# One change to a sparse-attention and feed-forward kernel: order of the block moves, early weight pieces, and who splits x

## The reference

```
scores = q @ k.T / 8 ; thresh = max(scores, row) - tau
scores = where(scores >= thresh, scores, -1e9)
attn = exp(scores - max) / (sum + 1e-9) ; x = attn @ v        # tokens x 512
h = x @ w_in ; g = max(h, 0) + alpha * min(h, 0) ; x = g @ w_out   # 512 -> 2048 -> 512
out = (((x @ w1) * (x @ w2)) @ w3) @ w_out2                    # 512 -> 1024 -> 1024 -> 512
```

## Time and profile before

| what | value |
|---|---|
| three runs, median (lowest to highest) | 1059.97 us (1058.85 to 1061.64) |
| the profiled execution, own time | 1060.03 us |
| its span in the profile | 1058.1 us |
| busy share PE / DVE / ACT / POOL | 94% / 49% / 40% / 45% |
| attention stage | to about 480 us |
| DMA engines, mean busy share of 150 to 200 us | 0.85 |

### The profile page before, as it was taken

One profiled execution on the slowest core, in us unless ns is written; L12 is line 12 of the kernel. 1 busy time (PEld: TensorE's weight loads), 2 busy tenths in 40 slices (PEclk: granted clock), 3 DMA queues, 4 the chain that ended last, 5 costly groups with the idle time before them and its releaser, 6 DMA issues.

```text
span 1058.1 us, 18205 instructions
## 1 busy us (share of the span) xinstructions
PE 990.3 (94%) x6848; PEld 899.6 (85%) x6848; DVE 519.6 (49%) x1374; ACT 420.0 (40%) x1000; POOL 472.2 (45%) x580
## 2 busy tenths in 40 slices
PE   3799956999999999999999999999999999999998
PEld 2566634777877787889999999999999999999998
DVE  6888977899998998922332222222111111111111
ACT  5666655666665666434323333333111111211210
POOL 5877768766666656323444444444212111111211
PEclk9799986999999999999999999999999999999999
DMA  7389898787878686768153222263211011011000
GB/s 261 86 242 276 263 302 199 197 229 185 234 196 237 184 208 181 198 168 300 56 198 131 113 112 113 112 250 133 91 68 45 24 68 46 23 68 46 24 23 24
DMA packets 53224, 156.39 MB, mean 148 GB/s; under 512 B 8208, under 2 KB 20496, under 8 KB 49424
## 3 DMA queue, kind: packets, MB, share of 16 engines
q1 hardware_dynamic: 42144, 122.78, 37.3%
q10 hardware_dynamic: 10992, 32.45, 10.8%
HBM read 79.05 MB, written 32.51 MB: 105 GB/s over the span
## 4 chain that ended last, share of the span: by engine, by line
PE 61%; DVE 13%; DMA 7%; POOL 5%; issue 5%; ACT 4%; SPq 4%; ACTq 1%; POOLq 0%
PE psum L693 19%; PE psum L726 19%; PE psum L679 11%; PE psum L638 5%; DVE nmx L940 5%; DMA zbuf<-ybuf 4%; DVE e_ring L953 4%; PE psum L600 3%; SPq L443 3%; POOL g L1069 2%; PE psum L651 2%; PE psum L583 2%; DVE g_raw L985 1%; ACT g_raw L840 1%; DMA k_raw<-k 1%
## 5 line engine op out<-in xcount | busy, mean ns | idle before, releaser
L1069 POOL TENSOR_TENSOR g<-g_raw,g 128x288 fp32r<-128x288 f32 x192 | 158.7, 831 | 378.8 <-ACT g L922 235.1
L726 PE MATMUL psum<-xy,w_a 128*128 128x288 f32 x1536 | 206.1, 295 | 0.6 <-DVE y_buf L1053 0.6
L726 PEld LDWEIGHTS psum<-xy,w_a 128*128 128x128 f32 x1536 | 205.2, 188 | 0.8 <-DVE y_buf L1053 0.8
L583 PE MATMUL psum<-ks,qs 128*128 128x288 f32 x640 | 121.4, 320 | 37.3 <-DVE e_ring L953 25.3
L583 PEld LDWEIGHTS psum<-ks,qs 128*128 128x128 f32 x640 | 101.2, 204 | 53.9 <-DVE e_ring L953 35.5
L1098 POOL TENSOR_SCALAR e_ring<-e_ring,rden,uni 128x576 f32<-128x576 f32 x144 | 118.6, 825 | 60.3 <-DVE rden L964 56.8
L805 ACT ACTIVATE e_ring<-psum,nmx 128x576 f32<-128x576 f32 x144 | 106.7, 741 | 82.1 <-DVE nmx L940 82.0
L985 DVE SCALAR_TENSOR_TENSOR g_raw<-g_raw,beta_sb,psum 128x288 f32<-128x288 f32 x128 | 65.7, 514 | 127.2 <-ACT g_raw L840 127.0
L953 DVE SCALAR_TENSOR_TENSOR e_ring<-psum,thr,e_ring 128x576 f32<-128x576 f32 x144 | 115.4, 801 | 12.4 <-ACT e_ring L805 11.9
L600 PE MATMUL psum<-zbuf,vs 128*64 128x320 f32 (+1 forms) x640 | 107.9, 433 | 13.7 <-DMA zbuf<-ybuf 10.9
L940 DVE TENSOR_REDUCE nmx<-psum 128x1 f32<-128x576 f32 x144 | 108.5, 753 | 22.7 <-PE psum L583 22.3
(11 more groups left out here) (53 smaller groups left out, 1105.7 us busy)
## 6 DMA issues: line engine op xcount, KB each, us to landing
zbuf<-ybuf SPq DMA_DIRECT2D x96, 180.0 KB, 4.4
raw_a<-weights SPq DMA_DIRECT2D x56, 256.0 KB, 6.9
zbuf<-ybuf SPq DMA_DIRECT2D x96, 144.0 KB, 4.3
xy<-xs SPq DMA_DIRECT2D x12, 1152.0 KB, 5.2
q_raw<-q ACTq DMA_DIRECT2D x16, 576.0 KB, 6.2
xs<-x_hl SPq DMA_DIRECT2D x32, 288.0 KB, 6.1
ys<-xy SPq DMA_DIRECT2D x8, 1152.0 KB, 4.4
xy<-ys SPq DMA_DIRECT2D x8, 1152.0 KB, 5.1
```

Source lines behind the costliest of these rows:

```text
L583: last = mm(dst, qs[:, par, at:at + P], ks[:, par, part, h, cols], start=(m == 0), stop=(m == 2 * len(terms) - 1))
L726: last = mm(psum[:, 2 * ab + f % 2, 0:CH], w_a[:, wp, slot, (f % 4) * P:(f % 4 + 1) * P], xy[c][:, xp, kt, :], start=(n == 0), stop=(n == ...
L1069: sub = lambda out_, a, hi: nc.gpsimd.tensor_tensor(out_, a, hi.bitcast(F32), ALU.subtract)
```

## The change

- SP issues its twelve moves at one step, 21 + 9n, by a fixed list that alternates between source partitions 0 to 63 and 64 to 127. ScalarE's four stay in their steps, two of each half, with other blocks.
- Pieces 24 to 31 ("parked") are loaded at steps 10 to 13 into memory of xy and g that nobody uses yet, each with a semaphore of its own; their hi copy waits for the product that frees their slot. Step 0 loads 6 pieces and not 16; the other 10 load at step 9 after k of pair 1 has landed. The last eight pieces before the fill are copied one step later.
- ScalarE copies x from PSUM as fp32 in the four parts, then makes hi from that in one copy of 128x576, after the exp of the second of the two steps; GpSimd subtracts once, 128x576, a step later. VectorE has no part in it. TensorE waits for the evacuation (`s_xe`), the store of x is one step later.
- In the first pair VectorE makes six low parts before its first row minimum and four after it. ScalarE asks for k of pair 1 in step 2 and for q in step 9.

```diff
+SP_MOVES = [(0, 0), (2, 2), (0, 1), (2, 3), (1, 0), (3, 2), (0, 2), (2, 0), (0, 3), (2, 1), (1, 1), (3, 3)]
+ACT_MOVES = [(1, 2), (1, 3), (3, 0), (3, 1)]
...
-PIECE_STEPS += [45, 46, 48, 49, 51, 52, 54, 55, 57, 58, 60, 61, 63, 64, 66, 67]
+PIECE_STEPS += [45, 46, 48, 49, 51, 52, 54, 55, 58, 59, 61, 62, 64, 65, 67, 68]
...
+FIRST_LOADS = 6
+def parked(k):
+    return N_WP <= k < N_WP + FT
...
 def load_step(k):
-    return 0 if k < 2 * FT else PRODUCT_STEPS[4 * product_before(k) + 3] + 2 + max(0, k - N_WP - FT) // 2
+    if parked(k):
+        return TILES + 1 + (k - N_WP) // 2
+    if k < 2 * FT:
+        return 0 if k < FIRST_LOADS else TILES
+    return PRODUCT_STEPS[4 * product_before(k) + 3] + 2 + max(0, k - N_WP - FT) // 2
...
+        with ExitStack() as place:
+            raw_xy = sb("raw_xy", [2 * KD * CH], F32, place)
+            raw_g = sb("raw_g", [2 * FT * CH], F32, place)
...
+        with ExitStack() as place:
+            raw_x = sb("raw_x", [2, 2, SEQ], F32, place)
         x_hl = sb("x_hl", [2, 2, SEQ], F32R, attn)
...
-            def move_blocks(n, y):
+            def move_blocks(n):
                 sp.wait_ge(s_t, TILES * (n + 1))
                 if n >= 1:
-                    sp.wait_ge(s_pv[y], n)
-                for k in range(QD):
-                    dst, src = move(n, 2 * y, (2 * y + k) % QD)
-                    sp.dma_start(dst, src).then_inc(s_z[y], 16)
...
+                    for y in range(2):
+                        sp.wait_ge(s_pv[y], n)
+                for a, c in SP_MOVES:
+                    sp.dma_start(*move(n, a, c)).then_inc(s_z[a // 2], 16)
...
+                if parked(j):
+                    sp.dma_start(raw_piece(j), weights[j]).then_inc(s_park[j - N_WP], 16)
+                    return
...
             def store_x(n):
-                sp.wait_ge(s_xl, X_PARTS * (n + 1))
+                sp.wait_ge(s_xl, n + 1)
...
+                if s == TILES:
+                    sp.wait_ge(s_k_in, 32)
                 for j in range(EARLY):
...
-                for y in range(2):
-                    if pair_at(s, LAG_MOVE + y) is not None:
-                        move_blocks(pair_at(s, LAG_MOVE + y), y)
-                if pair_at(s, LAG_X[1] + 1) is not None:
-                    store_x(pair_at(s, LAG_X[1] + 1))
+                if pair_at(s, LAG_MOVE) is not None:
+                    move_blocks(pair_at(s, LAG_MOVE))
+                if pair_at(s, LAG_X[1] + 2) is not None:
+                    store_x(pair_at(s, LAG_X[1] + 2))
...
                     if n >= 1:
-                        pe.wait_ge(s_xl, X_PARTS * n - 2 + 2 * y)
+                        pe.wait_ge(s_xe, X_PARTS * n - 2 + 2 * y)
...
             def early_hi(j):
-                act.wait_ge(s_w_in[slot], 16 * loads_into(j))
-                copy(w_a[:, 0, slot, :], raw_a[:, 1, slot, :]).then_inc(s_w_hi, 1)
+                piece_loaded(act, j)
+                if parked(j):
+                    act.wait_ge(s_wp, product_before(j) + 1)
+                copy(w_a[:, 0, slot, :], raw_piece(j)).then_inc(s_w_hi, 1)
...
-            def x_hi(n, part):
+            def x_out(n, part):
...
-                dst, src = x_piece(n, part)
-                copy(dst[0], src).then_inc(s_xh, 1)
+                copy(*x_piece(n, part)).then_inc(s_xe, 1)
+
+            def x_hi(n):
+                act.wait_ge(s_xe, X_PARTS * (n + 1))
+                copy(x_hl[:, n % 2, 0, :], raw_x[:, n % 2, 1, :]).then_inc(s_xh, 1)
...
                 if tile_at(s) is not None:
                     exp_of(tile_at(s))
+                if pair_at(s, LAG_X[1]) is not None:
+                    x_hi(pair_at(s, LAG_X[1]))
...
-                if s % TILES == 4 and s // TILES + 1 < NPAIR:
+                if s == 2:
+                    load_keys(1)
+                elif s % TILES == 4 and TILES < s < TILES * (NPAIR - 1):
                     load_keys(s // TILES + 1)
-                if s % TILES == 8 and s // TILES + 1 < NPAIR:
+                if s == LEAD:
+                    load_queries(1)
+                elif s % TILES == 8 and TILES < s < TILES * (NPAIR - 1):
...
-            def x_lo(n, part):
-                dve.wait_ge(s_xh, X_PARTS * n + 2 * (part // 2) + 2)
-                dst, src = x_piece(n, part)
-                sub(dst[1], src, dst[0]).then_inc(s_xl, 1)
...
                 if s == 2:
-                    for low in FIRST_LO:
+                    for low in FIRST_LO[:FIRST_KEYS]:
+                        first_lo(low)
...
+                if s == LEAD + 1:
+                    for low in FIRST_LO[FIRST_KEYS:]:
+                        first_lo(low)
...
+            def x_lo(n):
+                pool.wait_ge(s_xh, n + 1)
+                sub(x_hl[:, n % 2, 1, :], raw_x[:, n % 2, 1, :], x_hl[:, n % 2, 0, :]).then_inc(s_xl, 1)
...
+                if pair_at(s, LAG_X[1] + 1) is not None:
+                    x_lo(pair_at(s, LAG_X[1] + 1))
```

More of the change, by code:

```diff
@@ L161, in loads_into @@
 def loads_into(j):
-    return sum(early_slot(i) == early_slot(j) for i in range(j + 1))
+    return sum(early_slot(i) == early_slot(j) and not parked(i) for i in range(j + 1))
 def product_at(s):
@@ L312, in build @@
         s_pv = [sem(f"values_product_ready_{i}") for i in range(2)]
+        s_xe = sem("x_evacuated")
         s_xh = sem("x_hi_ready")
@@ L317, in build @@
         s_w_in = [sem(f"weight_piece_loaded_{i}") for i in range(SLOTS)]
+        s_park = [sem(f"parked_piece_loaded_{i}") for i in range(FT)]
         s_b_in = [sem(f"second_half_piece_loaded_{i}") for i in range(SLOTS)]
@@ L398, in x_rest @@
             src = psum[rows, 4 + h, 0:2 * (MAIN + 1) * SQ].rearrange("p (a c) -> p a c", a=2)
-            dst = [x_hl[rows, par, hl, MAIN * P:].rearrange("p (a i) -> p a i", a=2) for hl in range(2)]
+            dst = raw_x[rows, par, 1, MAIN * P:].rearrange("p (a i) -> p a i", a=2)
             return dst, src[:, :, 0:SQ] if h else src[:, :, MAIN * SQ:]
@@ L404, in x_half @@
             src = psum[:, 4 + y, 0:2 * (MAIN + 1) * SQ].rearrange("p (a t i) -> p t a i", a=2, t=MAIN + 1)
-            dst = [x_hl[:, par, hl, 0:MAIN * P].rearrange("p (t a i) -> p t a i", t=MAIN, a=QD)[:, :, 2 * y:2 * y + 2, :]
-                   for hl in range(2)]
+            dst = raw_x[:, par, 1, 0:MAIN * P].rearrange("p (t a i) -> p t a i", t=MAIN, a=QD)[:, :, 2 * y:2 * y + 2, :]
             return dst, src[:, y:y + MAIN, :, :]
@@ L415, in move, with raw_piece, piece_loaded @@
                     ybuf[a * SQ:(a + 1) * SQ, n % 2, FIRST[c]:FIRST[c + 1], :])
+        def raw_piece(j):
+            if not parked(j):
+                return raw_a[:, 1, early_slot(j), :]
+            at = (j - N_WP) % 4 * PC
+            return raw_xy[:, at:at + PC] if j < N_WP + 4 else raw_g[:, 4 * PC + at:4 * PC + at + PC]
+        def piece_loaded(eng, j):
+            if parked(j):
+                eng.wait_ge(s_park[j - N_WP], 16)
+            else:
+                eng.wait_ge(s_w_in[early_slot(j)], 16 * loads_into(j))
         def w_c_part(i, part):
@@ L435, in load_values @@
                 sp.dma_start(vs[:, par, :, :, :], v[n]).then_inc(s_v_in[par], 16)
-            def move_blocks(n, y):
+            def move_blocks(n):
                 sp.wait_ge(s_t, TILES * (n + 1))
                 if n >= 1:
-                    sp.wait_ge(s_pv[y], n)
-                for k in range(QD):
-                    dst, src = move(n, 2 * y, (2 * y + k) % QD)
-                    sp.dma_start(dst, src).then_inc(s_z[y], 16)
-                    if k % 2 == 1:
-                        dst, src = move(n, 2 * y + 1, (2 * y + 3 + k // 2) % QD)
-                        sp.dma_start(dst, src).then_inc(s_z[y], 16)
+                    for y in range(2):
+                        sp.wait_ge(s_pv[y], n)
+                for a, c in SP_MOVES:
+                    sp.dma_start(*move(n, a, c)).then_inc(s_z[a // 2], 16)
             def load_piece(j):
                 slot = early_slot(j)
+                if parked(j):
+                    sp.dma_start(raw_piece(j), weights[j]).then_inc(s_park[j - N_WP], 16)
+                    return
                 if product_before(j) is not None:
                     sp.wait_ge(s_wp, product_before(j) + 1)
-                sp.dma_start(raw_a[:, 1, slot, :], weights[j]).then_inc(s_w_in[slot], 16)
+                sp.dma_start(raw_piece(j), weights[j]).then_inc(s_w_in[slot], 16)
             def load_b_piece(slot):
@@ L465, in load_interleaved @@
                     sp.wait_ge(s_h, FT * ck)
+                else:
+                    sp.wait_ge(s_w_lo[0], N_WP + 4)
                 if ck % 2 == 0:
@@ L825, in store_y, with move_blocks @@
                 act.dma_start(yp[ck, :, m, :], g_raw[:, raw_y(m), :]).then_inc(s_ya_out[raw_y(m)], 16)
-            def move_blocks(n, y, half):
+            def move_blocks(n, m):
+                a, c = ACT_MOVES[m]
                 act.wait_ge(s_t, TILES * (n + 1))
                 if n >= 1:
-                    act.wait_ge(s_pv[y], n)
```

(21 more changed lines are left out.)

4 lines of the change are left out of this document (1 added, 3 removed).

## The result

The changed kernel takes 1107.95 us (median; 1104.05 to 1111.9) against 1059.51, a ratio of 1.045 with the interval 1.041 to 1.050: 48 us slower, where 1048 and at most 1068 had been forecast. Rival A, the slower one, had been worked out at 1101 and given 12%.

What follows compares the result with a forecast made beforehand. Waits were taken to bound the attention stage, with TensorE nearly full in pairs carrying feed-forward work. Savings of 6.1 + 3.3 + 2.2 + 1.8 + 1.0 less 3.0 gave 11.4 us off 1060.03, rounded to 1048 us; range 1038 to 1068.

Steps and rivals of the forecast that it cites:

- Rival A: Block moves of the two halves do not overlap, so TensorE waits for the first half: +41 us, 1101; chance 0.12.
- the rate of alternating moves: SP's queue: if halves overlap, 12 moves take 7.0 us at 0.58 each, the first half's 11 take 6.4.
- The sum: Whole kernel: the gains and losses of all parts together save 11.4 us, giving 1048.
- The landing: After SP's 11th move: 4.4 us at the median until the first half is there, 10.8 us in all.
- partial case B: Halves overlap partly, near 260 GB/s: first half 1.5 us late in eight pairs, 12 us lost, 1060; chance 0.18.
- ten full waits: In Rival A, TensorE idles 4.7 us in each of ten pairs whose four steps in between hold no hidden units.
- six of 1.1 us: In Rival A, the six other odd pairs, whose steps leave up to 14.3 us, lose 1.1 us each.
- Second half: Moves of the second half ready some 5 us sooner, so TensorE's waits go: 3.3 and 2.2 us saved.
- Parked pieces: ScalarE's 7.93 us wait for a weight piece goes; the 9.30 us gap falls to about 3.2, 6.1 us saved.
- Split of x: VectorE relieved at tiles 1 and 3: 1.8 us saved, but five long pairs lose 0.6 each, 3.0 us.
- First pair: Start of the kernel: second k load lands 2 to 3 us sooner; 1.0 us saved, bounds -2 and +3.
- The sign that was named: In the first pair, the tenth row minimum would come 1 us nearer to the first.

Runs made afterwards that it cites:

- e3: Only block moves between SBUF partitions, in eight phases varying halves, queues and sizes, without computing the output; alternating halves 252 GB/s, all partitions 410.
- e1: The changed kernel with SP's six moves of the first half ahead of its six of the second; 1048.7 us, ratio 0.990 to the kernel before.
- e8: e1 with the last four weight pieces and the first load of x into xy issued behind the moves of pair 4; 1053.9 us, ratio 0.994.
- e9: e8 with the load of the next pair's k two steps later, behind ScalarE's four moves; 1053.1 us, ratio 0.995.
- e6: e1 with the first pair's loads and low parts as in the kernel before; 1054.2 us, ratio 0.994.

## Why the prediction was wrong

- *Step that failed: the rate of alternating moves.* The sum took "If two halves in flight together overlap, SP's 12 moves go out at its own pace ... 12 take 7.0 us". SP's moves, 166 KB each on average, would go at about 286 GB/s by that, with ScalarE's on top. e3 shows 252 for all moves together and the kernel 227; eleven issues took 10.54 us, not 6.4. The landing was not at fault: 4.6 us, for 4.4 in the sum. The pace of 0.58 us came from the first two issues of a train, and twelve take 12.27 us. The text had put the deciding rate at 330 GB/s with the k load beside the moves and at 260 with half of it. The second figure is wrong by its own terms: 267 is what the moves need alone (2.32 MB in 8.7 us), and with half of the k load it is 300. It had no row with both halves in flight, and still gave the forecast nearly four times the chance of A. Its partial case B was set near 260 GB/s, almost what was measured, but priced at 1.5 us of lateness with a landing of 3.5, and without the k load. The measured lateness was 4.9 us in the pair shown, near A's 4.7.
- *A's account* holds in place and nearly in size. With T for the first move, it had the first half at T + 15.4 against a need at T + 10.7; the values product came at T + 15.1. Its ten full waits are all there, 5.4 us on average for 4.7. Of its six of 1.1 us one is 3.8 and five are missing: 58.3 us in all for 54. In part that is luck, since A had 206 GB/s and no overlap; there is some overlap, and the k load beside it comes to the same. Missing was the clock behind the waits, some 10 us; 1108 was measured for 1101.
- *Second half:* as forecast, its waits are gone in the changed kernel. That shows little, since TensorE has by then waited for the eleventh of SP's twelve moves.
- *Parked pieces:* the 7.93 us wait is gone (6.1 counted). Taking them out of e1 costs 0.3 points of the ratio, within the noise. In e1 two other gaps of 5.7 and 8.2 us between row minima stand instead, where TensorE waits 3.6 and 5.5 us for the first half of pairs 3 and 4 (0.7 and 1.3 in the kernel before). The second goes when the late loads are put behind the moves (e8, 0.3), the first when the k load goes later as well (e9). So both come from other loads beside the moves, which the sum had not looked at.
- *Split of x:* 1.8 won and 3.0 lost were counted. At tile 3 of pairs 2 to 5 the interval fell by 0.65 to 0.73 us (from 3.09 to 2.44 in pair 2), 2.75 in all: the upper bound of 2.7, where half had been counted. GpSimd's subtraction took 1.43 us, for the 1.42 estimated. Wrong was "In short pairs TensorE's work covers all of this" (0.8 to 1.4 us per short pair won), and the loss of the long pairs is 0.2 at tile 3 and 0.1 in the whole pair (28.5 us for 28.4), not 0.6: the forecast's 29.0 is not there. The reading from a TensorE busy share of 24.39 of 24.80 was the error: the same 170 products are busy for 24.41 us in one of the windows above and for 24.00 in the other, so a share near the full did not mean that nothing was to be won.
- *First pair:* 1.0 counted, bounds -2 to +3. The tenth row minimum is at 36.25, 2.2 us sooner than before. The sign that was named did not come, though: it stands 26.1 us behind the first one, for 24.7, as the first itself is 3.6 us sooner. Without this part (e6) the ratio is 0.4 points higher, within the noise.
- *The sum without the moves:* e1_first_half_first runs at 1048.7, the forecast's number, with errors of the single terms that cancel. That is luck, and it does not make the forecast right: the terms for moves were in it.

## What to carry to other kernels

When transfers with different deadlines share a queue, what counts is when the last byte of the first-needed group lands. An interleaving for bandwidth pays only if the rate rises by more than the bytes that it puts ahead. Here 11 moves of SP for 6 asked for much more than the 1.24 times that it gives, and a load on another queue was let in as well. Where such a rate decides the sign, and no row shows it, the end at which nothing is gained should not get the small chance; a kernel of transfers alone settles it in one run.

## What the runs showed of the hardware

All figures of moves are from the one execution of e3_move_rates. Moves that read partitions 0 to 63 run at 196 to 208 GB/s; 204 and 208 are for writing to the lower and to the upper half. Alternating halves, in one queue or in two, moves of 184 KB run at 252 to 254; in double size, 228. Over all partitions it is 410. The DMA engines show a busy share of 0.97 to 1.03 in all of these, so that share says nothing of how close the rate is to its limit.

In the changed kernel TensorE stood idle from 299.9 to 304.87 and then took up its products. Its granted clock was 1.00 until 304, 0.50 from 304.5 to 307.5 and 1.00 again from 308. Eight products that took 1.29 us at 2.4 GHz took 2.37 at 1.2.
